# Turning the keys of twelve items on VectorE instead of TensorE, and other small moves, in a gated linear attention with two MLPs

## What is computed

```python
f = 1.0 / (1.0 + np.exp(-f_logit))
for t in range(S):
    state = f[:, :, t, :, None] * state + np.einsum('bhd,bhe->bhde', k[:, :, t], v[:, :, t])
    y[:, :, t] = np.einsum('bhd,bhde->bhe', q[:, :, t], state)
# first MLP
h = x @ w_in
g = np.where(h >= 1, h, np.where(h <= -1, 0.0, (h + 1) ** 2 / 4.0))
x = g @ w_out
# second MLP
h = x @ w_in
P = a[0] + a[1] * h + a[2] * h**2 + a[3] * h**3
Q = 1.0 + np.abs(b[0]) * np.abs(h) + np.abs(b[1]) * h**2
out = (P / (Q + 1e-06)) @ w_out
```

## Time and profile before

| | us |
|---|---|
| median of 3 runs | 917.87 |
| lowest and highest | 916.12, 917.94 |
| the profiled execution, all of it | 915.96 |
| its span, first to last instruction | 914.2 |
| TensorE busy (matmuls) | 885.7 |
| VectorE busy | 664.8 |
| ScalarE busy | 632.0 |
| GpSimd busy | 277.8 |

### The profile page before, as it was taken

The page is one execution under the profiler, slowest core; times in us unless marked ns, Lnnn a source line. Parts: engine busy times, 40 slices in busy tenths (PEclk is TensorE's granted clock), DMA queues, the critical chain, the costliest instruction groups (busy, mean ns, idle before and its releaser), DMA issues.

```text
span 914.2 us, 13161 instructions
## 1 busy us (share of the span) xinstructions
PE 885.7 (97%) x4786; PEld 730.6 (80%) x4786; DVE 664.8 (73%) x813; ACT 632.0 (69%) x821; POOL 277.8 (30%) x202
## 2 busy tenths in 40 slices
PE   4899999999999999999999999999999999999997
PEld 3687778888888888888888887888888888888885
DVE  8876666566555666565344799999889889899884
ACT  5766665655566555655577888888787887887872
POOL 4445500000100000000055375634354244353233
PEclk9999999999999999999999999999999999999999
DMA  7643122112111311200224111001001001000001
GB/s 210 195 137 90 37 69 70 36 36 87 35 36 36 101 52 38 78 20 1 87 87 138 53 52 35 1 35 35 1 34 34 23 11 34 34 0 0 34 0 39
DMA packets 26744, 48.71 MB, mean 53 GB/s; under 512 B 4544, under 2 KB 7616, under 8 KB 26688
## 3 DMA queue, kind: packets, MB, share of 16 engines
q1 hardware_dynamic: 26688, 47.99, 17.2%
HBM read 36.18 MB, written 9.44 MB: 50 GB/s over the span
## 4 chain that ended last, share of the span: by engine, by line
PE 80%; DVE 9%; ACT 5%; issue 4%; POOL 1%; POOLq 0%; DMA 0%; DVEq 0%; SPq 0%; ACTq 0%
PE acc L1144 18%; PE acc L1188 18%; PE h_pair L1127 17%; PE at_pair L1166 10%; PE h_pair L1166 10%; PE at_pair L1067 2%; PE at_pair L1086 2%; DVE growth L844 2%; PE at_pair L1081 2%; DVE g L915 1%; POOL g_lo L544 1%; ACT t L647 1%; ACT t L644 1%; DVE guess L862 1%; DVE probs L883 1%
## 5 line engine op out<-in xcount | busy, mean ns | idle before, releaser
L544 POOL TENSOR_TENSOR g_lo<-g,g_hi 128x1024 fp32r<-128x1024 f32 x48 | 116.9, 2436 | 217.0 <-DVE t L944 212.5
L915 DVE SCALAR_TENSOR_TENSOR g<-h_pair,t 128x512 f32<-128x512 f32 x96 | 66.4, 691 | 136.9 <-ACT t L647 136.6
L644 ACT ACTIVATE t<-h_pair,half 128x512 f32<-128x512 f32 x96 | 66.0, 687 | 95.4 <-PE h_pair L1127 94.3
L509 POOL TENSOR_TENSOR k_s<-k_in,growth 128x512 f32<-128x512 f32 x22 | 29.6, 1346 | 286.8 <-DVE growth L844 270.0
L1188 PE MATMUL acc<-g_hi,w_hi 128*128 128x512 f32 x288 | 112.4, 390 | 1.9 <-POOL g_lo L544 1.9
L1127 PE MATMUL h_pair<-x_hi,w_hi 128*128 128x512 f32 x288 | 113.0, 392 | 1.0 <-DVE g L915 0.7
L1127 PE MATMUL h_pair<-x_hi,w_lo 128*128 128x512 f32 x288 | 112.2, 389 | 0.0
L1127 PE MATMUL h_pair<-x_lo,w_hi 128*128 128x512 f32 x288 | 112.1, 389 | 0.0
L1188 PE MATMUL acc<-g_lo,w_hi 128*128 128x512 f32 x288 | 112.1, 389 | 0.0
L1188 PE MATMUL acc<-g_hi,w_lo 128*128 128x512 f32 x288 | 112.1, 389 | 0.0
L654 ACT CAST g_hi<-g 128x512 fp32r<-128x512 f32 x88 | 54.6, 620 | 80.2 <-DVE g L915 80.2
(11 more groups left out here) (142 smaller groups left out, 2035.9 us busy)
## 6 DMA issues: line engine op xcount, KB each, us to landing
w_raw<-w SPq DMA_DIRECT2D x32, 384.0 KB, 3.8
f_in<-fC SPq DMA_DIRECT2D x48, 96.0 KB, 2.8
k_in<-kC SPq DMA_DIRECT2D x48, 96.0 KB, 2.4
q_in<-qC SPq DMA_DIRECT2D x48, 96.0 KB, 2.2
mlp_out<-o_sb SPq DMA_DIRECT2D x18, 256.0 KB, 3.0
x_raw<-mlp_out SPq DMA_DIRECT2D x6, 768.0 KB, 4.4
outT<-o_sb SPq DMA_DIRECT2D x18, 256.0 KB, 2.0
v_in<-vC SPq DMA_DIRECT2D x22, 192.0 KB, 2.5
```

The costliest lines, as they stand in the source:

```text
L544: nc.gpsimd.tensor_tensor(g2_lo[r][:, :, :], g2[r][:, :, :], g2_hi[r][:, :, :].bitcast(F32), ALU.subtract).then_inc(lo2_ready, 1)
L644: nc.scalar.activation(t1[n % 2][:, :], h1[n % 2], ACT.Relu, scale=0.5, bias=half[:, :]).then_inc(relu1_ready, 1)
L915: nc.vector.scalar_tensor_tensor(out=g1[n % 2][:, :], in0=h1[n % 2], scalar=1.0, in1=t1[n % 2][:, :], op0=ALU.max, op1=ALU.min).then_inc(g ...
```

## The change

For the items 8 to 19 (`turned(i)`) TensorE's transposes and ScalarE's copies go. VectorE transposes the scaled keys in blocks of 32 by 32 instead: one instruction takes 32 partitions and 4 x 32 columns to 32 other partitions, so 16 instructions for an item, in four strips of four. Strip 0 stands in stage 2 of the item before, behind `scale_queries`, strip 1 behind the low half of stage 3, strips 2 and 3 behind the low half of the item's own stage 1. The deltas wait for all 16, and for the state term of the item before, which the transposes waited for. There are two tiles `k_nat`, used in turn, and the waits of the copies are one item looser. GpSimd's `scale_keys` waits for the blocks instead of the transposes, two items back.

`states(i)` moves from stage 3 to stage 2, ahead of `rest_y`, `newton` and `scale_queries`. In the second MLP the low halves of the last two units are computed by VectorE: that of 46 between L940 and L944 of unit 47, that of 47 at the end, in two pieces of 512 columns, each behind its own piece of rounding.

```diff
-        k_nat = lay.tile("k_nat", NB)
+        k_nat = [lay.tile(f"k_nat{u}", NB) for u in range(2)]
...
+        def turned(i):
+            return 2 * GROUPS <= i < ITEMS - GROUPS
...
+        def tail(n):
+            return isinstance(n, int) and n >= N2 - 2
...
             def rational_lo(n, r):
+                if tail(n):
+                    return
...
             def copy_keys(i):
-                if i >= ITEMS - GROUPS:
+                if i >= ITEMS - GROUPS or turned(i):
                     return
-                if i > 0 and i != HEAD - 1:
-                    act.wait_ge(delta_ready, i)
+                if i == HEAD + 1:
+                    act.wait_ge(delta_ready, 2)
+                elif i >= 2 and i != HEAD - 1:
+                    act.wait_ge(delta_ready, i - 1)
...
+                if isinstance(n, int) and n == N2 - 1:
+                    for c in range(UW):
+                        nc.scalar.copy(g2_hi[r][:, c, :], g2[r][:, c, :]).then_inc(hi2_ready, 1)
+                    return
...
+            def turn_keys(i, strips):
+                if i >= ITEMS or not turned(i):
+                    return
+                dve.wait_ge(k_ready, i + 1)
+                dve.wait_ge(delta_ready, i - 1)
+                for q in strips:
+                    src = k_scaled(i)[q * SQ:(q + 1) * SQ, :].rearrange("p (b t) -> p b t", b=BATCH)
+                    for j in range(CK // SQ):
+                        dst = k_natural(i)[j * SQ:(j + 1) * SQ, :].rearrange("p (b t) -> p b t", b=BATCH)
+                        nc.vector.transpose(dst[:, :, q * SQ:(q + 1) * SQ], src[:, :, j * SQ:(j + 1) * SQ]).then_inc(turned_keys, 1)
...
+            def tail_lo(n):
+                r, lasts = n % R2, n == N2 - 1
+                dve.wait_ge(multiplied2, n - R2 + 1)
+                if not lasts:
+                    dve.wait_ge(hi2_ready, n + 1)
+                    nc.vector.tensor_tensor(g2_lo[r][:, :, :], g2[r][:, :, :], g2_hi[r][:, :, :].bitcast(F32),
+                                            ALU.subtract).then_inc(tail_lo_ready, 1)
+                    return
+                for c in range(UW):
+                    dve.wait_ge(hi2_ready, n + 1 + c)
+                    nc.vector.tensor_tensor(g2_lo[r][:, c, :], g2[r][:, c, :], g2_hi[r][:, c, :].bitcast(F32),
+                                            ALU.subtract).then_inc(tail_lo_ready, 1)
...
-                if stage == 3:
-                    if i % GROUPS != LAST:
-                        rest_y(i)
-                    states(i)
+                if stage == 3 and i % GROUPS != LAST:
+                    rest_y(i)
                 spline_join(n)
                 if stage == 0:
                     mask(i)
                 spline_lo(n)
                 if stage == 0:
                     scan(i + 1)
+                if stage == 1:
+                    turn_keys(i, (2, 3))
                 if stage == 2:
+                    states(i)
                     if i % GROUPS == LAST:
                         rest_y(i)
                     newton(i + 1)
                     scale_queries(i + 1)
+                    turn_keys(i + 1, (0,))
+                if stage == 3:
+                    turn_keys(i + 1, (1,))
...
             def transposes(i):
-                if i >= ITEMS - GROUPS:
+                if i >= ITEMS - GROUPS or turned(i):
                     return
...
-                pe.wait_ge(knat_ready, i + 1)
+                if turned(i):
+                    pe.wait_ge(turned_keys, 16 * (i + 1 - 2 * GROUPS))
+                    pe.wait_ge(delta_done, 2 * i)
+                else:
+                    pe.wait_ge(knat_ready, i + 1)
...
+                    if isinstance(n, int) and n == N2 - 1 and o == 0:
+                        pe.wait_ge(tail_lo_ready, c + 2)
```

More of the change, by code:

```diff
@@ L14 @@
 HS = 64
+SQ = 32
 PAIRS = BATCH * HEADS // 2
@@ L226, in build @@
         knat_ready = sem("knat_ready")
+        turned_keys = sem("turned_keys")
         delta_ready = sem("delta_ready")
@@ L269, in build @@
         lo2_ready = sem("lo2_ready")
+        tail_lo_ready = sem("tail_lo_ready")
         multiplied2 = sem("multiplied2")
@@ L287, in k_natural @@
         def k_natural(i):
-            return k_nat_head if i == HEAD - 1 else k_nat
+            return k_nat_head if i == HEAD - 1 else k_nat[i % 2]
+        def turned(i):
+            return 2 * GROUPS <= i < ITEMS - GROUPS
         def values(i):
@@ L507, in scale_keys @@
                     pool.wait_ge(scores_ready, before + 1)
-                    pool.wait_ge(kt_ready, min(before + 1, ITEMS - GROUPS))
+                    if before >= 2 * GROUPS:
+                        pool.wait_ge(turned_keys, 16 * (min(before + 1, ITEMS - GROUPS) - 2 * GROUPS))
+                    else:
+                        pool.wait_ge(kt_ready, before + 1)
                 nc.gpsimd.tensor_tensor(k_scaled(i)[:, :], k_in[u][:, :], growth[u][:, :], ALU.mult).then_inc(k_ready, 1)
@@ L941, in rational_step @@
                                                    op0=ALU.add, op1=ALU.mult).then_inc(e_done, 1)
+                if tail(n - 2):
+                    tail_lo(n - 2)
                 if have2(n - 1):
@@ L1033, in _ @@
             run2(dve, rational_step, 2 + R2, UNITS + 1)
+            tail_lo(N2 - 1)
             dve.wait_ge(flag_set, 1)
@@ L1171, in rational_second @@
             def rational_second(n, m, blk):
-                pe.wait_ge(lo2_ready, n + 1)
+                if not tail(n):
+                    pe.wait_ge(lo2_ready, n + 1)
+                elif n == N2 - 2:
+                    pe.wait_ge(tail_lo_ready, 1)
                 if isinstance(n, int) and n < UNITS and blk == 0:
```

## The result

| | before | after |
|---|---|---|
| median, lowest and highest of the timed runs, us | 917.31 (916.06 to 918.51; 17 runs) | 919.57 (917.87 to 921.57; 17 runs) |
| the profiled execution: all of it, its span | 915.96, 914.2 | 918.9, 917.2 |

The ratio of after to before is 1.003, with a 95% interval of 1.0022 to 1.0037: the change makes the kernel slower by 0.3%, 2.3 us. The forecast was 918.0 us, with 0.36 each for faster and for no change and 0.28 for slower.

A forecast was written before the change was run, and what follows sets the result against it. TensorE, busy 97% of the span, was taken to bound the kernel. Item 8 (12d - 1.68), eleven items (8d - 2.61 each) and the tail (-2.0) gave +0.1 us, so 918.0 us; range 911.8 to 926.0, the forecast's own 916.1 to 919.7.

The forecast's parts named there:

- d: Time from start to start of one VectorE block transpose, taken as 0.325 us, bounds 0.205 and 0.49 us.
- long blocks: Rival: blocks slower, from d = 0.342, deltas wait longer, 1.0 us for every 10 ns; chance 0.28.
- The transposes, 0.44 us an item: TensorE's step to the scores falls from 0.76 to 0.32 us, 5.3 us for twelve items.
- The block's time, d = 0.325 us: VectorE's block of 128 elements: 0.298 us long plus 0.027 us spacing, without overlap.
- both rivals on d: Blocks short or overlapping (d 0.205 to 0.306, 1.8 to 6.1 us faster), chance 0.28; or long (from 0.342), chance 0.28.
- A steady item, 8d - 2.61: Each of eleven items: deltas wait 8d - 2.17 = 0.43 us, taking back the 0.44 us saved; -0.01 us.
- Item 8, 12d - 1.68: First turned item: VectorE comes late from items 5 to 7, deltas wait 12d - 1.18 us; +2.2 us.
- The entry costs nothing: Rival: VectorE catches up before item 8's deltas; -2.7 us from whatever d gives, 915.3 us; chance 0.08.
- The tail: Last units: VectorE takes GpSimd's low halves, so unit 47 starts at 903.55 instead of 905.54; -2.0 us.
- The moved state terms: Items 6 and 7: transposes' waits go, scores wait instead, VectorE's sum unchanged; costed at nothing, else -1 us.
- The wait as its own price: TensorE's waits before the deltas were costed by length: 8d - 2.17 us in a steady item, 12d - 1.18 in item 8.

The follow-up runs named there:

- after_states_late: The changed kernel with the state terms put back behind the rest of y in stage 3; turning and tail stay: 918.60 us, ratio 1.0023 to the kernel before.
- turning_only: The kernel before with only the keys of items 8 to 19 turned on VectorE; state terms and tail as before: 920.97 us, ratio 1.0045.
- turn_from_9: As after_states_late, but only items 9 to 19 turned on VectorE, item 8 transposed by TensorE: 914.61 us, ratio 0.998 to the kernel before.
- fill_8: As after_states_late, with twelve more TensorE products, overwritten later, in front of item 8's deltas: 917.39 us, ratio 1.0011 to the kernel before.
- states_early_only: The kernel before with the state terms moved ahead of newton and nothing else: 919.46 us, ratio 1.0031.
- tail_only: The kernel before with only VectorE computing the low halves of units 46 and 47: 913.86 us, ratio 0.9972.
- the blocks in the gaps: As turn_from_9, with six blocks an item put where VectorE waits for ScalarE's rounding between join and low half: 909.41 us, ratio 0.9922 to the kernel before.

## Why the prediction was right or wrong

**The median** (918.0 forecast, 919.57 measured) lies in the range, and even in the forecast's own, 916.1 to 919.7. That is luck in part: these bounds were made from d alone, and what moved the time was a term that had no bounds. Against before the forecast was +0.1 us, no change that could be told, and the measured change is +2.3 us, clear of noise. I had 0.28 for slower, and gave it to long blocks, which didn't come. Step by step:

- *The transposes, 0.44 us an item*: right (0.76 to 0.32 us; -0.46 an item where nothing waits).
- *The block's time, d = 0.325 us*: right, 302 ns long and 0.329 to 0.335 us apart. The copy and the price of an element carried it; both rivals on d fell. The Trainium skill's figure (VectorE: DVE Perf Modes, The three transpose paths) of 311 ns is for bf16 and 128 partitions; a block of f32 on 32 partitions with as many columns took 302 ns.
- *A steady item, 8d - 2.61 = -0.01 us*: right, 0.0 measured in after (0.03 in `after_states_late` and `turning_only`, 0.06 in `turn_from_9`, 0.12 in `fill_8`); the wait 0.42 us from start to start against 0.43.
- *Item 8, 12d - 1.68 = +2.2 us*: right in size. The wait was 2.55 us against 2.7; from unit 8 to 20 after lost 4.34 us, of which `states_early_only` has 2.12, which leaves 2.2; `fill_8` shows 2.07. "The entry costs nothing" fell.
- *The tail, -2.0 us*: right in the traces, with unit 47 at 903.51 against 903.55.
- *The moved state terms, "I cost it at nothing"*: this is the step that failed, **+2.1 us**. The prediction saw that VectorE sets the pace there, and then took its sum as fixed ("since VectorE's sum is the same"). The instructions were the same, their lengths not: what stood outside GpSimd's splitting was pushed under it, 1.06 us in each of the items 5 and 6. Its own words on item 8 named that splitting as what slows the scans. The bound of this term should have gone up to what newton's two free steps can grow by: 0.68 and 0.69 us became 1.23 and 1.11, 0.97 us an item.
- *The wait as its own price*: the prediction priced a wait by its length. Where it is long the half clock comes on top. In after this did not change the sum, but it decides the parts: item 8 alone cost 4.9 us with late state terms, and undoing the early state terms won at most 0.7 us by the ratios (1.0023 against 1.003, the intervals overlap) where it should have won 2.1.

The sum of the prediction with the failed term put right is 0.1 + 2.1 = +2.2 us; measured by the medians, +2.3.

**Not settled.** Why of waits of nearly one length one is followed by the half clock and the other not (2.31 and 2.38 us in after; 1.67 us in `tail_only` and 1.64 us in before, at the same place in the same code). Why `turn_from_9` loses 0.3 us at its first item and 0.2 at the first item of two blocks. Whether item 8 can be turned at a gain with the blocks in the gaps wasn't tried. That GpSimd's splitting lengthens newton is read from the rows and from a move that puts one beside the other; no run took the splitting away. Item 8's share in after is worked out from runs with the state terms early and late, not from one that changes it alone.

## What to carry to other kernels

When work moves from the bounding engine to one that has idle time, ask where in its chain each piece stands: in front of a step that waits for a third engine anyway it is free, in front of a step with no idle time before it, it is paid in full and may cost more than was saved. An instruction moved past others also moves them; look at what the engine beside it does at their new time, for the sum of an engine's lengths isn't kept. And price a long wait of TensorE with the half clock that may follow it.

## What the hardware showed that was not expected

- Behind a wait of 3.21 us TensorE's clock fell to 1.2 GHz for about 6 us, which cost 2.9 us on top of the wait; twelve products of no use in its place (3.02 us) kept the clock up and gave this back, 1.9 us of it to the end of the turned items.
- Executions whose code is the same up to there differ in the first 30 us: behind the wait at 23.8 us the clock fell in four of ten (waits of 1.8 to 2.3 us, the others 1.0 to 1.7), and the first unit started 0.6 to 1.6 us later in these.
- VectorE's products with two SBUF inputs took 1.10 to 1.23 us beside GpSimd's splitting instead of 0.69; the rest of y, with an input in PSUM, took 1.40 us for two beside it and 1.41 without. Which of the two grows went by which started first: a VectorE step that began 0.01 us ahead of a piece of the splitting kept its 0.69 us, and that piece took 1.28 us instead of 0.74.
